# Window attention and two feed-forward layers: chunk 1's first unit is handled ahead of the copies of chunk 0's sums, and softmax work moves to other steps

## The chip, the cores and the metric

The kernel runs on one core of a Trainium2 chip. The metric is device time in microseconds (us) of one execution, as the median of several. Five engines work side by side and wait for one another by semaphores: TensorE (PE in the rows; PEld is its weight loads) multiplies, VectorE (DVE), ScalarE (ACT) and GpSimd (POOL) work element by element, and SyncE (SP) starts most DMAs.

## The reference, cut to what matters

```python
w = softmax(weight_gen)                     # over 7 taps, for 8 heads at each of 2 x 4096 tokens
out = einsum('bshk,bskhg->bshg', w, x_unf)  # each token: 7 rows of x, weighted per head of 24
h = out.reshape(8192, 192) @ w_in1          # 192 x 2048
g = h * cos(h);  y = g @ w_out1             # 2048 x 192
h2 = y @ w_in2;  g2 = maximum(0.01 * h2, h2)
return g2 @ w_out2
```

Products are in fp32 quality: every operand is split in a high part (rounded by a copy) and a low part (the rest, by a subtraction), and TensorE sums high x high, high x low and low x high.

## The kernel before

The 8192 tokens are worked in 16 chunks of 512. Iteration `i` (0 to 16) computes the first layer of chunk `i` and the second layer of chunk `i - 1`, in 18 steps. The 2048 hidden columns are taken in 8 units of 256 for each layer: `FIRST_UNITS` stand in steps 0 to 7, `SECOND_UNITS` in steps 8, 9, 10, 11, 12, 14, 15 and 17. Steps 13 and 16 have no unit. In this text unit (i, q) is unit q (0 to 15) of iteration i; q 0 to 12 stand in the step of the same number, q 13 in step 14, q 14 in step 15 and q 15 in step 17 (so q 8 to 12 are steps 8 to 12).

Of one unit of the first layer: TensorE fills a PSUM slot (`slot0` to `slot2`, by step modulo 3); ScalarE rounds it to whole turns (`whole`, L791); VectorE makes the fraction (L1017); ScalarE takes the sine (L832); VectorE multiplies (L1043, `g_ready`); ScalarE copies the high part (`g_hi`, L732, `hi_ready`); VectorE subtracts (`g_lo`, L919, `lo_ready`); and TensorE adds the unit's second product to `acc_a` and `acc_b`. Of a unit of the second layer ScalarE makes `gate` from the slot (L795) and `g_hi`, and VectorE only `g_lo`.

TensorE's order is fixed: `both_products(i, q, j, r)` fills unit (i, q) and, three units behind, sums unit (j, r). Its first ten half matmuls are of the filling alone; then it waits for `lo_ready` of the unit to be summed. The filling of unit (i, 0) reads the chunk's input: `x1_a_hi` in the first two terms, `x1_a_lo` in the third, `x1_b` (both halves) in the fourth, and `x1_up` in the fifth. It is done beside the sum of unit (i - 1, 13).

ScalarE and VectorE each run `step_of(i, step)` for every step. In a step the high part and the low part of the unit of the step before are taken (`pending_high`, `pending_low`). In step 16 `split_high` and `split_low` make the next chunk's input from `x_raw_a` and `x_raw_b`: `x1_a_hi` (L743) and `x1_b`'s upper half (L745) on ScalarE, `x1_a_lo` (L931) and `x1_b`'s lower half (L934) on VectorE; `x1_up` is a copy on ScalarE (L755) up to chunk 2 and on GpSimd (L659) from chunk 3 on. After the last unit of a layer the sums are copied out of PSUM: in step 0 of iteration 1 for chunk 0, otherwise in step 9, by `leave_mid_a` on ScalarE (L759) and `leave_mid_b` on VectorE (fold L948, `mid_b` L953).

Between these stand the attention of the next chunk (on VectorE in steps 7 to 11, `ATT_AT`) and the softmax of chunks further ahead. The softmax of a group of chunks is max, subtract, exponentials, sum, guard, invert, multiply: the exponentials are on ScalarE (`EXP_AT`, L855), the rest on VectorE (`SOFT_AT`, L1068 to L1083). Exponentials and sine need different tables, so each `exponentials` and each `load_sine` in the loop comes with an `ACT_TABLE_LOAD`. They stand in iterations 1, 3 and 5.

GpSimd makes the low parts of the second layer's weights once: `in_a_lo` in two pieces (L686), `in_b_lo` (L691) and `out_hi_lo` in eight (L697). It starts on them when the multiply of softmax part 2 is done (`soft_count(2, "multiply")`).

## Time and profile before

| what | before |
|---|---|
| median of 3 runs | 1150.26 us (1150.2 to 1150.3) |
| profiled execution, its own time | 1151.76 us |
| span of the profiled execution, first to last instruction | 1150.0 us |
| TensorE busy | 1132.5 us (98%) |
| VectorE busy | 934.6 us (81%) |
| ScalarE busy | 724.9 us (63%) |
| GpSimd busy | 87.1 us (8%) |
| granted TensorE clock, mean | 0.997 |

The profile lists the instructions of one execution with start and length, what ended each engine's idle time, and a chain of work followed back from the last instruction. A number in brackets behind a row is idle time ahead of it, and the name behind the arrow is what ended it. Since matmuls are pipelined, one is 0.39 us long while the next starts 0.23 us behind it.

### The profile page before, as it was taken

Reading aid. Unit: us, or ns where it says so; the run is one execution under the profiler, and the core shown is the slowest. Engines: PE = TensorE matmul, PEld = TensorE weight load, DVE = VectorE, ACT = ScalarE, POOL = GpSimd, SP = SyncE. Lnnn points to the kernel's source line nnn. Section 1 sums busy time; section 2 is a strip of 40 time slices with the busy share of each in tenths; the row PEclk is TensorE's granted clock in tenths of the full one; section 3 lists DMA queues with packets and bytes.
Section 4 is the critical chain, followed back from the end, with each engine's and each line's share of the span. In section 5 each row is a group of like instructions: output and inputs, shape, how many; then the busy total and the mean of one; then the engine's idle time right before and its main releaser. Section 6 shows DMA issues by size and latency. Waiting matters only on the chain.

```text
span 1150.0 us, 22937 instructions
## 1 busy us (share of the span) xinstructions
PE 1132.5 (98%) x9766; PEld 996.1 (87%) x9766; DVE 934.6 (81%) x913; ACT 724.9 (63%) x775; POOL 87.1 (8%) x80
## 2 busy tenths in 40 slices
PE   7999999999999999999999999999999999999998
PEld 5778989988888888899998989988888898898976
DVE  7989798888979889697896978969798796978543
ACT  5666774766747666575665757566575665757544
POOL 5870000000000000000000000000000000000000
PEclk9999999999999999999999999999999999999999
DMA  9760201103011020201102011020201102010001
GB/s 257 203 129 1 63 2 32 45 1 77 1 37 41 1 76 1 54 24 31 47 1 76 1 36 42 4 74 1 47 31 30 48 1 77 1 37 7 1 15 29
DMA packets 85262, 48.41 MB, mean 42 GB/s; under 512 B 58156, under 2 KB 78762, under 8 KB 84776
## 3 DMA queue, kind: packets, MB, share of 16 engines
q1 hardware_dynamic: 80712, 41.70, 14.1%
q0 software_dynamic: 4448, 5.24, 2.5%
q8 instruction: 77, 1.26, 0.4%
q14 instruction: 25, 0.20, 0.1%
HBM read 35.12 MB, written 11.80 MB: 41 GB/s over the span
## 4 chain that ended last, share of the span: by engine, by line
PE 89%; DVE 4%; ACT 1%; issue 1%; ACTq 0%; DVEq 0%
PE slot L1200 41%; PE acc_a L1200 28%; PE acc_b L1200 18%; DVE g_lo L919 1%; DVE prods L327 0%; DVE prods L318 0%; ACT g_hi L732 0%; DVE gate L1017 0%; PE acc_b L1173 0%; ACT gate L795 0%; ACT L855 0%; PE acc_b L1174 0%; PE acc_a L1166 0%; PE acc_a L1165 0%; ACT taps_w L855 0%
## 5 line engine op out<-in xcount | busy, mean ns | idle before, releaser
L1200 PE MATMUL acc_a<-g_hi,out_hi_lo 64*128 64x512 f32 x2000 | 699.0, 390 | 0.0
L919 DVE TENSOR_TENSOR g_lo<-gate,g_hi 128x1024 fp32r<-128x1024 f32 x252 | 309.2, 1227 | 119.0 <-ACT g_hi L732 118.5
L1200 PE MATMUL acc_b<-g_hi,out_hi_lo 64*128 64x512 f32 x1000 | 389.6, 390 | 5.7 <-DVE g_lo L919 3.0
L1200 PEld LDWEIGHTS acc_a<-g_hi,out_hi_lo 64*128 64x128 f32 x2000 | 370.0, 185 | 26.6
L1200 PE MATMUL acc_a<-g_lo,out_hi_lo 64*128 64x512 f32 x1000 | 387.9, 388 | 0.0
L1200 PE MATMUL acc_b<-g_lo,out_hi_lo 64*128 64x512 f32 x1000 | 387.6, 388 | 0.0
L732 ACT ACTIVATE g_hi<-gate 128x1024 fp32r<-128x1024 f32 x252 | 267.3, 1061 | 97.4 <-PE acc_b L1200 78.0
L1200 PE MATMUL slot<-x_a_hi,in_a_lo 64*128 64x512 f32 x1024 | 301.8, 390 | 1.3 <-DVE g_lo L919 0.6
L1200 PE MATMUL slot<-x_a_lo,in_a_hi 64*128 64x512 f32 x1024 | 300.9, 388 | 0.4 <-DVE x_a_lo L938 0.4
L1200 PE MATMUL slot<-x_b,in_b_hi 64*128 64x512 f32 x1024 | 300.9, 388 | 0.2 <-DVE x_b L941 0.2
L1200 PE MATMUL slot<-x_a_hi,in_a_hi 64*128 64x512 f32 x1024 | 300.7, 388 | 0.0
L795 ACT ACTIVATE gate<-slot 128x1024 f32<-128x1024 f32 x128 | 130.8, 1022 | 125.4 <-PE slot L1200 99.0
L1200 PEld LDWEIGHTS acc_b<-g_hi,out_hi_lo 64*128 64x128 f32 x1000 | 184.9, 185 | 24.8 <-issue 8.9
L1200 PEld LDWEIGHTS acc_a<-g_lo,out_hi_lo 64*128 64x128 f32 x1000 | 185.3, 185 | 12.1
L1200 PEld LDWEIGHTS acc_b<-g_lo,out_hi_lo 64*128 64x128 f32 x1000 | 185.0, 185 | 10.4
L1017 DVE SCALAR_TENSOR_TENSOR gate<-slot,whole 128x1024 f32<-128x1024 f32 x127 | 155.1, 1221 | 46.8 <-ACT whole L791 46.1
L791 ACT ACTIVATE whole<-slot 128x1024 int32<-128x1024 f32 x127 | 130.1, 1024 | 72.7 <-PE slot L1200 72.7
L1200 PEld LDWEIGHTS slot<-x_a_hi,in_a_lo 64*128 64x128 f32 x1024 | 145.9, 185 | 17.4 <-PE slot L1200 2.9
L1200 PEld LDWEIGHTS slot<-x_a_lo,in_a_hi 64*128 64x128 f32 x1024 | 146.1, 185 | 13.2 <-DVE x_a_lo L938 0.8
L1200 PEld LDWEIGHTS slot<-x_b,in_b_hi 64*128 64x128 f32 x1024 | 146.1, 185 | 13.0 <-DVE x_b L941 1.0
L1200 PEld LDWEIGHTS slot<-x_a_hi,in_a_hi 64*128 64x128 f32 x1024 | 146.1, 185 | 12.0
L1043 DVE SCALAR_TENSOR_TENSOR gate<-slot,gate 128x1024 f32<-128x1024 f32 x124 | 151.6, 1222 | 6.0 <-ACT gate L832 4.1
(110 smaller groups left out, 1023.0 us busy)
## 6 DMA issues: line engine op xcount, KB each, us to landing
x_win<-in_x SPq DMA_DIRECT2D x14, 960.0 KB, 4.7
x_columns<-prods SPq DMA_DIRECT2D x56, 96.0 KB, 2.0
out<-turned_a SPq DMA_DIRECT2D x240, 16.0 KB, 1.5
x_raw_a<-x_columns SPq DMA_DIRECT2D x14, 256.0 KB, 2.8
out<-turned_b SPq DMA_DIRECT2D x120, 16.0 KB, 1.5
result<-x_columns SPq DMA_DIRECT2D x14, 128.0 KB, 3.0
out_raw<-in_moe_w_out SPq DMA_DIRECT2D x3, 512.0 KB, 8.6
out_hi_lo<-in_moe_w_out POOLq DMA_DIRECT2D x2, 768.0 KB, 10.7
```

What stands on the lines that cost most here:

```text
L732: nc.scalar.activation(g_hi[:, q % 2, :], result_of(i, q), ACT.Copy)\
L791: nc.scalar.activation(whole[:, q % 2, :], slot, ACT.Identity, bias=0.25)\
L795: nc.scalar.activation(gate[:, q % 2, :], slot, ACT.Prelu, alpha=0.01)\
L919: nc.vector.tensor_tensor(g_lo[:, q % 2, :], result_of(i - b, q), g_hi[:, q % 2, :].bitcast(FP32), ALU.subtract)\
L1017: nc.vector.scalar_tensor_tensor(gate[:, q % 2, :], slot, 0.25, whole[:, q % 2, :], ALU.add, ALU.subtract)\
L1043: nc.vector.scalar_tensor_tensor(result_of(i, q), slot, RADIANS, gate[:, q % 2, :], ALU.mult, ALU.mult)\
L1200: return nc.tensor.matmul(to, w[rows, :], x[rows, :], start=start, stop=stop)
```

## The change

- `SOFT_AT` and `EXP_STEP`, `SINE_STEP`: max and subtract of a group stand together in step 12 (before: step 8 of iteration 1, and steps 13 and 14 of iterations 2 and 4). The exponentials stand in step 13 (before 10) and the sine's table load in step 14 (before 12) of iterations 1, 3 and 5. Sum, guard and invert stand in step 16 (before: sum in 13, guard and invert in 14), and the multiply in step 17 (before 16).
- The sum, guard, invert and multiply of part 2 move from step 9 of iteration 0 to step 0 of iteration 1, behind the fraction of unit (1, 0).
- In step 0 of iteration 1, VectorE's product of unit (1, 0) comes ahead of fold and `mid_b`, and its `g_lo` right behind them, ahead of the fraction of unit (1, 1). ScalarE's `g_hi` of unit (1, 0) comes ahead of `mid_a` and of `whole` of unit (1, 1).
- GpSimd starts on the second layer's weights when `g_lo` of unit (1, 0) is done.

```diff
--- before.py
+++ after.py
@@ -432,18 +432,16 @@
             yield (b_lows(W1.in_b_lo, cols), b_lows(W1.in_b_lo_raw, cols),
                    b_pairs(W1.in_b_hi, cols).bitcast(FP32))
 
-        EXP_STEP, SINE_STEP = 10, 12
+        EXP_STEP, SINE_STEP = 13, 14
         HEAD_ROWS, SOFT_ROWS = [[slice(a * J * heads, b * J * heads) for a, b in chunks]
                                 for chunks in (SOFT_HEADS, SOFT_CHUNKS)]
 
 
-        SOFT_AT = {(0, 9): [(2, part) for part in TAIL_PARTS]}
+        SOFT_AT = {}
         for n, (begin, end) in enumerate(((1, 1), (2, 3), (4, 5)), 2):
-            SOFT_AT[begin, 8 if n == 2 else 13] = [(n, "max")]
-            SOFT_AT.setdefault((begin, 8 if n == 2 else 14), []).append((n, "subtract"))
-            SOFT_AT[end, 13] = [(n + 1, "sum")]
-            SOFT_AT[end, 14] = [(n + 1, "guard"), (n + 1, "invert")]
-            SOFT_AT[end, 16] = [(n + 1, "multiply")]
+            SOFT_AT[begin, 12] = [(n, "max"), (n, "subtract")]
+            SOFT_AT[end, INPUT_STEP] = [(n + 1, "sum"), (n + 1, "guard"), (n + 1, "invert")]
+            SOFT_AT[end, INPUT_STEP + 1] = [(n + 1, "multiply")]
         EXP_AT, SINE_AT = [[(i, step) for i in (1, 3, 5)] for step in (EXP_STEP, SINE_STEP)]
 
         def softmax_operands(rows):
@@ -679,7 +677,7 @@
                 .then_inc(w2_hi_loaded[2], 16)
 
 
-            pool.wait_ge(soft, soft_count(2, "multiply"))
+            pool.wait_ge(lo_ready, unit(1, 0) + 1)
             pool.wait_ge(w2_loaded[0], 16)
             pool.wait_ge(w2_hi_loaded[0], 16)
             for cols in W2_PIECES:
@@ -734,7 +732,7 @@
 
             def pending_high(i, step):
                 b, prev = back(step, 1)
-                if is_unit(i - b, prev):
+                if (i, step) != (1, 1) and is_unit(i - b, prev):
                     high_part(i - b, UNITS.index(prev))
 
             def split_high(i, step, chunk):
@@ -831,6 +829,9 @@
                     act.wait_ge(fraction, first_units(i, q))
                     nc.scalar.activation(gate[:, q % 2, :], gate[:, q % 2, :], ACT.Sin,
                                          scale=TURN).then_inc(cos_ready, 1)
+                if (i, step) == (1, 0):
+
+                    high_part(1, 0)
                 j = first_out(i, step)
                 if j is not None:
                     act.wait_ge(summed, unit(j, 7) + 1)
@@ -901,9 +902,21 @@
 
         @block.vector
         def _(dve):
+            def product(i, q):
+                slot = slots[UNITS[q] % SLOTS][:, :, :].rearrange("p a n -> p (a n)")
+                dve.wait_ge(cos_ready, first_units(i, q))
+                nc.vector.scalar_tensor_tensor(result_of(i, q), slot, RADIANS, gate[:, q % 2, :],
+                                               ALU.mult, ALU.mult).then_inc(g_ready, 1)
+
+            def low_part(i, q):
+                dve.wait_ge(hi_ready, unit(i, q) + 1)
+                nc.vector.tensor_tensor(g_lo[:, q % 2, :], result_of(i, q),
+                                        g_hi[:, q % 2, :].bitcast(FP32), ALU.subtract)\
+                    .then_inc(lo_ready, 1)
+
             def pending_low(i, step):
                 b, prev = back(step, 1)
-                if is_unit(i - b, prev):
+                if (i, step) != (1, 1) and is_unit(i - b, prev):
                     q = UNITS.index(prev)
                     if unit(i - b, q) == 0:
                         dve.wait_ge(unit_act, 3)
@@ -915,10 +928,7 @@
                                                 g_hi[:, 0, N:].bitcast(FP32), ALU.subtract)\
                             .then_inc(lo_ready, 1)
                         return
-                    dve.wait_ge(hi_ready, unit(i - b, q) + 1)
-                    nc.vector.tensor_tensor(g_lo[:, q % 2, :], result_of(i - b, q),
-                                            g_hi[:, q % 2, :].bitcast(FP32), ALU.subtract)\
-                        .then_inc(lo_ready, 1)
+                    low_part(i - b, q)
 
             def split_low(step, chunk):
                 slot = slots[step % SLOTS]
@@ -1023,6 +1033,12 @@
                     for instruction in of_chunk_1[ATT_POOL + 1:]:
                         instruction()
                 pending_low(i, step)
+                if (i, step) == (1, 0):
+
+
+                    for part in TAIL_PARTS:
+                        softmax(2, part)
+                    product(1, 0)
                 j = first_out(i, step)
                 if j is not None:
                     if j >= 1:
@@ -1038,11 +1054,10 @@
                         nc.vector.scalar_tensor_tensor(result_of(i, q)[:, cols], slot[:, cols], RADIANS,
                                                        gate[:, 0, cols], ALU.mult, ALU.mult)\
                             .then_inc(done, 1)
-                elif in_first:
-                    dve.wait_ge(cos_ready, first_units(i, q))
-                    nc.vector.scalar_tensor_tensor(result_of(i, q), slot, RADIANS,
-                                                   gate[:, q % 2, :], ALU.mult, ALU.mult)\
-                        .then_inc(g_ready, 1)
+                elif in_first and (i, step) != (1, 0):
+                    product(i, q)
+                if (i, step) == (1, 0):
+                    low_part(1, 0)
                 if i < LAST:
                     split_second_low(i, step)
                 if step == TURN_STEP and i >= 2:
```

VectorE at the start of iteration 1, before. The softmax rows are part 2's, `slot0` holds unit (1, 0) and `slot1` unit (1, 1):

```order
L1074 TENSOR_REDUCE scratch<-taps_w 128x32
L1077 TENSOR_SCALAR scratch<-scratch 128x32
L1080 RECIPROCAL scratch<-scratch 128x32
L1083 TENSOR_TENSOR taps_w<-taps_w,scratch 128x224
L1017 SCALAR_TENSOR_TENSOR gate<-slot0,whole 128x1024
L948 COPY fold<-acc_b 64x512
L953 TENSOR_TENSOR mid_b<-acc_b,fold 64x512
L1043 SCALAR_TENSOR_TENSOR gate<-slot0,gate 128x1024
L1017 SCALAR_TENSOR_TENSOR gate<-slot1,whole 128x1024
L919 TENSOR_TENSOR g_lo<-gate,g_hi 128x1024
L1043 SCALAR_TENSOR_TENSOR gate<-slot1,gate 128x1024
```

The same place now (the fraction is L1027, the product L908, `g_lo` L913):

```order
L1027 SCALAR_TENSOR_TENSOR gate<-slot0,whole 128x1024
L1089 TENSOR_REDUCE scratch<-taps_w 128x32
L1092 TENSOR_SCALAR scratch<-scratch 128x32
L1095 RECIPROCAL scratch<-scratch 128x32
L1098 TENSOR_TENSOR taps_w<-taps_w,scratch 128x224
L908 SCALAR_TENSOR_TENSOR gate<-slot0,gate 128x1024
L958 COPY fold<-acc_b 64x512
L963 TENSOR_TENSOR mid_b<-acc_b,fold 64x512
L913 TENSOR_TENSOR g_lo<-gate,g_hi 128x1024
L1027 SCALAR_TENSOR_TENSOR gate<-slot1,whole 128x1024
L908 SCALAR_TENSOR_TENSOR gate<-slot1,gate 128x1024
```

The fraction moved ahead of the four softmax rows, the product ahead of the fold, and `g_lo` ahead of the next unit's fraction.

ScalarE at the same place, before; `g_hi` is that of unit (1, 0):

```order
L791 ACTIVATE whole<-slot0 128x1024
L832 ACTIVATE gate<-gate 128x1024
L759 ACTIVATE mid_a<-acc_a 128x512
L791 ACTIVATE whole<-slot1 128x1024
L732 ACTIVATE g_hi<-gate 128x1024
```

And now:

```order
L789 ACTIVATE whole<-slot0 128x1024
L830 ACTIVATE gate<-gate 128x1024
L730 ACTIVATE g_hi<-gate 128x1024
L757 ACTIVATE mid_a<-acc_a 128x512
L789 ACTIVATE whole<-slot1 128x1024
```

`g_hi` moved ahead of `mid_a` and of the next unit's `whole`.

ScalarE in iteration 3, before, from `gate` of unit (3, 11) on. `taps_w` is the exponentials, `spare` the sine's table load, the three `g_hi` are those of units (3, 10), (3, 11) and (3, 12):

```order
L795 ACTIVATE gate<-slot2 128x1024
L855 ACT_TABLE_LOAD
L855 ACTIVATE taps_w<-taps_w 128x1120
L732 ACTIVATE g_hi<-gate 128x1024
L795 ACTIVATE gate<-slot0 128x1024
L732 ACTIVATE g_hi<-gate 128x1024
L850 ACT_TABLE_LOAD
L850 ACTIVATE spare<-ident 1x1
L732 ACTIVATE g_hi<-gate 128x1024
```

And now, from `gate` of unit (3, 12) on; the two `g_hi` in one row are those of (3, 11) and (3, 12), the one behind `spare` is that of (3, 13):

```order
L793 ACTIVATE gate<-slot0 128x1024
L730 ACTIVATE g_hi<-gate 128x1024 x2
L793 ACTIVATE gate<-slot2 128x1024
L856 ACT_TABLE_LOAD
L856 ACTIVATE taps_w<-taps_w 128x1120
L793 ACTIVATE gate<-slot0 128x1024
L851 ACT_TABLE_LOAD
L851 ACTIVATE spare<-ident 1x1
L730 ACTIVATE g_hi<-gate 128x1024
L741 ACTIVATE x1_a_hi<-x_raw_a 128x512
L743 ACTIVATE x1_b<-result 64x512
```

Both table loads and the exponentials moved from ahead of `g_hi` of (3, 10) and (3, 12) to ahead of `g_hi` of (3, 13), behind which stands the next chunk's input.

## Rows read from the trace of the kernel before

**Rows 1.** The page: busy time by engine (first line), and the chain that ended last.
```profile
PE 1132.5 (98%) x9766; PEld 996.1 (87%) x9766; DVE 934.6 (81%) x913; ACT 724.9 (63%) x775; POOL 87.1 (8%) x80
...
PE 89%; DVE 4%; ACT 1%; issue 1%; ACTq 0%; DVEq 0%
```

**Rows 2.** Timeline of TensorE: start, length, instruction, idle before and what ended it.
```profile
74.74 0.50 PE L1200 MATMUL acc_b<-g_hi,out_hi_lo 64*128 64x512 f32 x1 [1.77 <-DVE g_lo L919]
...
85.12 0.39 PE L1200 MATMUL acc_b<-g_hi,out_hi_lo 64*128 64x512 f32 x1
...
111.86 0.47 PE L1200 MATMUL acc_b<-g_hi,out_hi_lo 64*128 64x512 f32 x1 [0.71 <-DVE mid_b L953]
...
263.87 0.50 PE L1200 MATMUL acc_b<-g_hi,out_hi_lo 64*128 64x512 f32 x1 [0.38 <-DVE g_lo L919]
```

**Rows 3.** Waits of TensorE: in total, how many times, the longest.
```profile
PE acc_b L1200 <- DVE g_lo L919: 3.0, 4, 1.8
```

**Rows 4.** Windows: length, busy times, granted clock, DMA share, GB/s.
```profile
75.10:78.60 3.50, 3.50 (x20) 2.76 (x18) 3.50 (x4) 2.12 (x2) 3.50 (x4) 0.51 0.01 2
```

**Rows 5.** Timeline of VectorE at the start of iteration 1.
```profile
64.98 0.38 DVE L1074 TENSOR_REDUCE scratch<-taps_w 128x32 f32<-128x224 f32 x1
...
66.31 1.22 DVE L1017 SCALAR_TENSOR_TENSOR gate<-slot,whole 128x1024 f32<-128x1024 f32 x1
68.56 0.69 DVE L948 COPY fold<-acc_b 64x512 f32<-64x512 f32 x1 [1.03 <-PE acc_b L1200]
69.29 0.68 DVE L953 TENSOR_TENSOR mid_b<-acc_b,fold 64x512 f32<-64x512 f32 x1
...
72.23 2.46 DVE L919 TENSOR_TENSOR g_lo<-gate,g_hi 128x1024 fp32r<-128x1024 f32 x1
```

**Rows 6.** Timeline of ScalarE at the start of iteration 1.
```profile
64.25 1.03 ACT L791 ACTIVATE whole<-slot 128x1024 int32<-128x1024 f32 x1 [0.44 <-PE slot L1200]
67.57 1.06 ACT L832 ACTIVATE gate<-gate 128x1024 f32<-128x1024 f32 x1 [2.29 <-DVE gate L1017]
69.46 0.60 ACT L759 ACTIVATE mid_a<-acc_a 128x512 f32<-128x512 f32 x1 [0.83 <-PE acc_a L1200]
69.95 1.02 ACT L791 ACTIVATE whole<-slot 128x1024 int32<-128x1024 f32 x1
```

**Rows 7.** Timeline of GpSimd on the second layer's weights.
```profile
66.49 4.76 POOL L686 TENSOR_TENSOR in_a_lo<-in_a_raw,in_a_hi 128x1024 fp32r<-128x1024 f32 x2 [5.08 <-DVE taps_w L1083]
71.22 2.39 POOL L691 TENSOR_TENSOR in_b_lo<-in_b_lo_raw,in_b_hi 128x1024 fp32r<-128x1024 f32 x1
```

**Rows 8.** Timeline of TensorE: filling of unit (2, 0), then of unit (3, 0).
```profile
133.11 0.40 PE L1200 MATMUL slot<-x_b,in_b_hi 64*128 64x512 f32 x2
...
202.02 0.42 PE L1200 MATMUL slot<-x_a_lo,in_a_hi 64*128 64x512 f32 x2
202.25 0.42 PE L1200 MATMUL slot<-x_b,in_b_hi 64*128 64x512 f32 x2
```

**Rows 9.** Timeline of ScalarE: iteration 1, iteration 2 (no exponentials), iteration 3.
```profile
124.04 1.06 ACT L732 ACTIVATE g_hi<-gate 128x1024 fp32r<-128x1024 f32 x1 [0.69 <-PE acc_b L1200]
...
193.25 1.06 ACT L732 ACTIVATE g_hi<-gate 128x1024 fp32r<-128x1024 f32 x1 [3.24 <-PE acc_b L1200]
...
199.04 0.62 ACT L745 ACTIVATE x_b<-result 64x512 fp32r<-64x512 f32 x1
...
255.49 1.14 ACT L855 ACTIVATE taps_w<-taps_w 128x1120 f32<-128x1120 f32 x1
...
260.93 1.28 ACT L850 ACT_TABLE_LOAD   x1
262.22 0.20 ACT L850 ACTIVATE spare<-ident 1x1 f32<-1x1 f32 x1
```

**Rows 10.** Timeline of VectorE: the input of chunk 3, in iteration 2.
```profile
200.00 1.10 DVE L931 TENSOR_TENSOR x_a_lo<-x_raw_a,x_a_hi 128x512 fp32r<-128x512 f32 x1
201.13 0.68 DVE L934 TENSOR_TENSOR x_b<-result,x_b 64x512 fp32r<-64x512 f32 x1
```

## The prediction

> **What bounds the kernel now.** The page comes first: TensorE is busy for 1132.5 of 1150.0 us, and 89% of the chain that ended last is its matmuls [rows 1]. So an edit elsewhere is worth what it takes from TensorE's waits, or adds to them. The second view is TensorE's timeline, read for idle time. A matmul of 0.39 us is followed by the next after 0.23 [rows 8], so a wait shown as idle costs 0.16 more than its figure. Behind the start-up four waits are within the change's reach: 1.77 ahead of the sum of unit (1, 0), 0.71 ahead of that of (1, 8), and 0.38 ahead of (3, 11) and again ahead of (5, 11) [rows 2, 3]. They cost 1.93, 0.87 and twice 0.54. The third view is the clock: in the 3.5 us behind the longest wait the granted clock was half [rows 4]. Its price is read from the sums: (1, 0) starts at 74.74 and (1, 2) at 85.12 [rows 2], 10.38 for two units. A unit otherwise takes 4.32, since the filling of (2, 0) and that of (3, 0) lie 69.14 apart for 16 units [rows 8]. So half clock cost 1.75. All that the change can win is 1.93 + 1.75 + 0.87 + 1.08 = 5.6 us, 0.5%.
>
> **The start of iteration 1.** I follow the new order with old lengths; what follows without a wait starts 0.07 to 0.10 before its predecessor's shown end, and a semaphore takes 0.03 to 0.05. `whole` of (1, 0) ends at 65.28 as before [rows 6]. VectorE's fraction now comes first: 65.31 to 66.53. The four softmax instructions took from 64.98 to about 66.40 [rows 5], 1.42 us, so now 66.45 to 67.87; the sine (1.06 [rows 6]) ends at 67.63, hidden by them. The product runs from 67.78 to 68.99, fold and `mid_b` (0.69 and 0.68 [rows 5]) to 70.32. ScalarE's `g_hi` runs from 69.03 to 70.09, and VectorE's `g_lo` from 70.25 to 71.47. TensorE asks for it at 74.74 - 1.93 = 72.81. So the wait is gone with 1.3 us to spare, and the half clock behind it with it. `mid_a` and `mid_b` are 0.5 and 0.35 us later, which nobody waits for before 72.8.
>
> What is late next is unit (1, 1). `mid_a` and `whole` of (1, 1) stand behind `g_hi`: `whole` ends at 71.51 (before 70.97 [rows 6]). Fraction to 72.76, sine to 73.86, product to 75.11, `g_hi` to 76.21, `g_lo` from 76.24 to 77.46. TensorE wants to sum it at 72.81 + 4.31 = 77.12 and starts at 77.51, a new wait of 0.39. The sum of (1, 2) then starts at 81.82 instead of 85.12: **3.3 us won**. Behind that VectorE needs some 3.5 us a unit (a fraction, a `g_lo`, a product) against TensorE's 4.31, and catches up.
>
> **GpSimd behind it.** Its first three pieces take 2.37, 2.37 and 2.39 us [rows 7]. The trace shows what they do to VectorE: `g_lo` of (1, 0), asked for at 72.23, took 2.46 instead of 1.22, as it began only about when GpSimd's `in_b_lo` ended (71.22 + 2.39 = 73.61, less 0.14); fraction and product, which read PSUM, were not slowed [rows 5, 7]. Now GpSimd starts at 71.56, so the third piece would start at 71.56 + 4.73 = 76.29, and the second lets go at about 76.20. VectorE asks for `g_lo` of (1, 1) at 76.24, between the two. I take it that it goes first, by 0.05 us, and GpSimd waits. The weights end some 6 us later than before, far ahead of unit (1, 8), the first to need them; the eight short pieces of `out_hi_lo` can hold up a `g_lo` by at most one piece, against a lead that has grown again.
>
> The Trainium skill says the same of this pair (SBUF — State Buffer, Who interferes with whom): whichever of the two starts first holds the shared ports for its whole instruction and the other blocks fully, and a VectorE instruction with one SBUF input is not touched. The rows above agree. It makes the whole stake a full piece.
>
> **Softmax out of step 8.** Without max and subtract ahead of it, chunk 1's fold waits for TensorE alone, and the sum of (1, 8) no longer for `mid_b`: 0.87 won. In step 12 of iterations 1, 2 and 4 the two lie ahead of a `g_lo` whose `g_hi` comes later anyway: nothing.
>
> **Exponentials out of step 10.** The waits at (3, 11) and (5, 11) came from ScalarE's table load and exponentials ahead of `g_hi` of (i, 10), with the attention's last steps pushed back behind it. Iteration 2 has no exponentials and no wait there. So 2 x 0.54 = 1.08 won.
>
> **Exponentials in step 13.** Here lies the price. I take iteration 2 as the pattern and put the new instructions in. `g_hi` of (i, 12) cannot start before TensorE ends a sum: 193.25 [rows 9]. Then come `gate` (to 195.24), table load 1.28, exponentials 1.14 (to 197.66), `gate` of the next unit (to 198.60), table load 1.28 and 0.20 (to 200.11) [rows 9], `g_hi` of (i, 13) (200.16 to 201.22), `x1_a_hi`, and `x1_b` (to 202.30, where the pattern has 199.66). On VectorE `g_lo` of (i, 13) runs from 201.25 to 202.48, `x1_a_lo` to 203.08, `x1_b` to 203.79. TensorE wants `x1_b` in the fourth term of the filling of (i + 1, 0), at 202.25 [rows 8]: in the pattern it was there at 201.81 [rows 10], 0.44 ahead. Now TensorE starts it at 203.84, **1.6 us late**. GpSimd's copy of `x1_up` starts at about the moment when VectorE asks for `x1_a_lo`, as in the pattern, where that took 1.10 instead of 0.68 [rows 10]: 0.4 more, 2.0 in all, in iterations 3 and 5. Without the copy it would be 1.6, and I take 2.0, since one of the two must wait. In iteration 1 the same chain starts at 124.04 [rows 9]; its exponentials are shorter (672 elements of 1120, an estimate of 0.75 us) and there is no GpSimd copy: `x1_b` at 124.04 + 10.54 - 0.39 = 134.19, wanted at 133.11 [rows 8]: 1.1 late.
>
> **Sums in steps 16 and 17.** In the pattern's lengths they fill VectorE's idle time behind `g_lo` of (i, 14) and make the first fraction of the next iteration about 1 us late, against a lead of over 1.5 us at the sum that needs it: nothing. Cover gone, it would be some tenths.
>
> **Sum.** -3.3 - 0.87 - 1.08 + 1.1 + 2 x 2.0 = -0.15 us. Against the profiled execution's 1151.76 that is 1151.6; the median of the runs is 1150.26, so **1150.1 us**. Why the profiled execution is 1.5 above the median no row says. If its half-clock stretch is not in the other runs, the gain there is 1.75 smaller and the time 1151.9, still no change that a measurement can tell (0.2% or 2.3 us).
>
> **Rivals.**
> 1. *GpSimd gets the ports first (slower).* VectorE's request at 76.24 and GpSimd's next piece at 76.29 are 0.05 apart, and each time is a sum of some eight lengths known to 0.01 or 0.02. From a request 0.05 later on, `g_lo` of (1, 1) waits for the third piece: 76.29 + 2.39 - 0.14 + 1.22 = 79.76. TensorE stands for 2.7 us, more than at the old wait, and half clock follows as in rows 4: the sum of (1, 2) starts at 85.9 instead of 81.8. 4.1 us more, 1154.2; without half clock 1152.4.
> 2. *A new wait halves the clock.* The waits of 2.0 us in iterations 3 and 5 are as long as the old one of 1.93, behind which the clock fell, but parted in two (for `x1_a_lo` and for `x1_b`) with matmuls between; the wait of 0.87 did not lower it. 1.75 for each: 1151.9 or 1153.6. The Trainium skill (TensorE: Matmul & The Clock Gate, HAM oscillation) lays a fall to idle gaps longer than any here; by that rule neither the old wait nor the new ones would cost clock, which rows 4 contradict for the old.
> 3. *The waits in steps 16 stay small (faster).* If ScalarE's chain were shorter than its parts, or the input's low parts came ahead of VectorE's `g_lo`, the price would be a third: 1145 to 1147.
> 4. *The change doesn't take effect at (1, 0).* Were something else late there, fold above all, the 3.3 us would stay: 1153.4. The fold needs only 69.6 against 72.8; small.
>
> **How the numbers follow.** Forecast 0.47, rival 1 0.24, rival 2 0.12 (two thirds of it one fall, within 0.2%), rival 3 0.14, rival 4 0.03. The forecast's own range is 1148.5 to 1152.0. Faster by over 0.2%: 0.15. Slower by over 0.2%: rival 1 nearly whole, part of 2, rival 4 and the forecast's upper edge, 0.34. Within: 0.51. The range leaves out the far half of rival 3 and rival 1's upper end: 1147.0 to 1154.5.
>
> **What would show it.** Right: no idle ahead of the sum of (1, 0) and no half clock behind it; 0.4 us ahead of (1, 1); no waits at (1, 8), (3, 11), (5, 11); waits named after `x_a_lo` and `x_b` of the input, 1.1 us in iteration 1 and 2.0 in 3 and 5. Rival 1: `g_lo` of (1, 1) shown with over 3 us, and GpSimd's pieces unbroken. Rival 2: half clock near 134, 270 or 410. Wrong: waits at the input under 0.5 us, or a wait elsewhere in iterations 1 to 5.

## The result, and the profile of the changed kernel

| what | before | changed |
|---|---|---|
| median of 20 runs each, side by side | 1150.53 us (1149.69 to 1151.78) | 1152.39 us (1151.08 to 1155.47) |
| ratio | | 1.0015, interval 1.0009 to 1.0022 |
| profiled execution, its own time | 1151.76 us | 1151.52 us |
| span | 1150.0 us | 1149.7 us |

The changed kernel is slower by 1.86 us. That is inside the band of 0.2% and inside the range, but it can be told from no change, and the forecast was a gain of 0.15. The two profiled executions alone would say that it is 0.24 faster. Both facts have to be explained. Three executions of the old kernel beside the experiments were disturbed (1414.57, 2335.8 and 6518.82 us) and stand in no median or range below.

In the listings below the lines have moved: the matmul is L1215, the fraction L1027, the product L908, `g_lo` L913, fold and `mid_b` L958 and L963, `x_a_lo` and `x_b` of the input L941 and L944, the table loads L856 and L851. The page shows the same bound as before (busy time by engine, then the chain that ended last):

```profile
PE 1132.5 (99%) x9766; PEld 940.0 (82%) x9766; DVE 936.7 (81%) x913; ACT 723.7 (63%) x775; POOL 87.5 (8%) x80
...
PE 88%; DVE 4%; ACT 2%; issue 2%; ACTq 0%; DVEq 0%
```

Four lines of TensorE's waits (total, times, longest), where [rows 3] had 3.0, 4, 1.8 for `g_lo`:

```profile
PE slot L1215 <- DVE x_a_lo L941: 2.2, 3, 0.9
...
PE acc_b L1215 <- DVE g_lo L913: 1.2, 3, 0.5
...
PE slot L1215 <- DVE x_b L944: 0.6, 3, 0.2
PE acc_b L1215 <- DVE mid_b L963: 0.6, 1, 0.6
```

TensorE's timeline has where they stand: the sum of (1, 0), now without a wait; the sums of (1, 1), (1, 4) and (1, 8); the input of chunk 2, and that of chunk 4:

```profile
71.75 0.39 PE L1215 MATMUL acc_b<-g_hi,out_hi_lo 64*128 64x512 f32 x1
...
76.53 0.49 PE L1215 MATMUL acc_b<-g_hi,out_hi_lo 64*128 64x512 f32 x1 [0.30 <-DVE g_lo L913]
...
90.11 0.50 PE L1215 MATMUL acc_b<-g_hi,out_hi_lo 64*128 64x512 f32 x1 [0.37 <-DVE g_lo L913]
...
108.25 0.46 PE L1215 MATMUL acc_b<-g_hi,out_hi_lo 64*128 64x512 f32 x1 [0.58 <-DVE mid_b L963]
...
129.81 0.50 PE L1215 MATMUL slot<-x_a_lo,in_a_hi 64*128 64x512 f32 x2 [0.38 <-DVE x_a_lo L941]
130.52 0.50 PE L1215 MATMUL slot<-x_b,in_b_hi 64*128 64x512 f32 x2 [0.21 <-DVE x_b L944]
...
270.06 0.51 PE L1215 MATMUL slot<-x_a_lo,in_a_hi 64*128 64x512 f32 x2 [0.94 <-DVE x_a_lo L941]
270.77 0.50 PE L1215 MATMUL slot<-x_b,in_b_hi 64*128 64x512 f32 x2 [0.21 <-DVE x_b L944]
```

From start to start, less the 0.23 of a matmul, these cost 0.45, 0.53, 0.73, 0.54 + 0.48 and 1.10 + 0.48; chunk 6 repeats chunk 4 with 1.57. The waits at (3, 11) and (5, 11) are gone. The clock stayed full where [rows 4] had 0.51 (window: length, busy times, granted clock, DMA share, GB/s):

```profile
70.00:73.50 3.50, 3.50 (x34) 2.87 (x32) 2.37 (x3) 2.21 (x3) 2.89 (x2) 1.00 1.11 171
```

VectorE's timeline at the start of iteration 1 answers [rows 5]: `g_lo` of (1, 0) takes 1.21 where it took 2.46, and that of (1, 1) 1.29.

```profile
64.26 1.23 DVE L1027 SCALAR_TENSOR_TENSOR gate<-slot,whole 128x1024 f32<-128x1024 f32 x1 [0.25 <-ACT whole L789]
...
66.73 1.22 DVE L908 SCALAR_TENSOR_TENSOR gate<-slot,gate 128x1024 f32<-128x1024 f32 x1
...
69.31 1.21 DVE L913 TENSOR_TENSOR g_lo<-gate,g_hi 128x1024 fp32r<-128x1024 f32 x1
...
72.83 1.23 DVE L908 SCALAR_TENSOR_TENSOR gate<-slot,gate 128x1024 f32<-128x1024 f32 x1 [1.13 <-ACT gate L830]
...
75.18 1.29 DVE L913 TENSOR_TENSOR g_lo<-gate,g_hi 128x1024 fp32r<-128x1024 f32 x1
```

**Where the time went.** The same fillings of a slot, set side by side in the two traces, give the balance. A profiled execution differs from another before the change begins: the filling that starts at 24.11 in the old kernel starts at 23.06 in the new one, where nothing was changed. Less this 1.05, the new kernel is ahead (-) or behind (+):

| stretch | forecast | measured |
|---|---|---|
| (1, 0) and (1, 1), with the half clock | -3.3 | -3.10 |
| (1, 4) | 0 | +0.65 |
| (1, 8) | -0.87 | -0.12 |
| input of chunk 2 | +1.1 | +1.07 |
| iterations 3 and 5 together | +2.92 | +2.40 |
| the rest | 0 | -0.12 |
| sum | -0.15 | +0.78 |

So in this pair the change costs 0.8 and not nothing. Another 1.1 us lies between this pair and the medians. A part of it is the half clock at (1, 0), which this profile of the old kernel had in full and many of its executions have not, as the experiments show. How large that part is stays open.

### The profile page after: what moved, and what is told of

Its sections match the earlier page's. It is cut to its first block, busy times and chain, and to the rows that moved or that the text cites. A ratio compares the mean times of both kernels' runs of the same rounds, so it can differ in the third digit from the quotient of the medians.

```text
span 1149.7 us, 22937 instructions
## 1 busy us (share of the span) xinstructions
PE 1132.5 (99%) x9766; PEld 940.0 (82%) x9766; DVE 936.7 (81%) x913; ACT 723.7 (63%) x775; POOL 87.5 (8%) x80
## 4 chain that ended last, share of the span: by engine, by line
PE 88%; DVE 4%; ACT 2%; issue 2%; ACTq 0%; DVEq 0%
PE slot L1215 41%; PE acc_a L1215 27%; PE acc_b L1215 18%; DVE g_lo L913 2%; DVE gate L1027 1%; ACT gate L793 0%; ACT L851 0%; DVE prods L318 0%; PE acc_b L1188 0%; ACT g_hi L730 0%; ACT taps_w L856 0%; DVE x_a_lo L941 0%; PE acc_a L1181 0%; PE acc_b L1189 0%; PE acc_a L1180 0%
## 5 line engine op out<-in xcount | busy, mean ns | idle before, releaser
L1215 PE MATMUL acc_a<-g_hi,out_hi_lo 64*128 64x512 f32 x2000 | 697.1, 388 | 0.0
L913 DVE TENSOR_TENSOR g_lo<-gate,g_hi 128x1024 fp32r<-128x1024 f32 x252 | 309.9, 1230 | 124.4 <-ACT g_hi L730 124.2
L1215 PEld LDWEIGHTS acc_a<-g_hi,out_hi_lo 64*128 64x128 f32 x2000 | 368.6, 184 | 36.0
L1215 PE MATMUL acc_b<-g_hi,out_hi_lo 64*128 64x512 f32 x1000 | 388.6, 389 | 3.8 <-issue 2.0
L1215 PE MATMUL acc_a<-g_lo,out_hi_lo 64*128 64x512 f32 x1000 | 387.0, 387 | 0.0
L1215 PE MATMUL acc_b<-g_lo,out_hi_lo 64*128 64x512 f32 x1000 | 386.9, 387 | 0.0
L1215 PE MATMUL slot<-x_a_lo,in_a_hi 64*128 64x512 f32 x1024 | 296.6, 387 | 2.2 <-DVE x_a_lo L941 2.2
L1215 PE MATMUL slot<-x_a_hi,in_a_lo 64*128 64x512 f32 x1024 | 297.7, 389 | 1.0 <-DVE g_lo L913 0.7
L1215 PE MATMUL slot<-x_b,in_b_hi 64*128 64x512 f32 x1024 | 296.7, 388 | 0.9 <-DVE x_b L944 0.6
L1215 PE MATMUL slot<-x_a_hi,in_a_hi 64*128 64x512 f32 x1024 | 296.3, 387 | 0.0
L1215 PEld LDWEIGHTS acc_b<-g_hi,out_hi_lo 64*128 64x128 f32 x1000 | 184.2, 184 | 28.4 <-issue 9.0
L1215 PEld LDWEIGHTS acc_a<-g_lo,out_hi_lo 64*128 64x128 f32 x1000 | 184.4, 184 | 17.5
L1215 PEld LDWEIGHTS acc_b<-g_lo,out_hi_lo 64*128 64x128 f32 x1000 | 184.4, 184 | 16.6
L1027 DVE SCALAR_TENSOR_TENSOR gate<-slot,whole 128x1024 f32<-128x1024 f32 x127 | 155.1, 1221 | 41.1 <-ACT whole L789 40.3
L1215 PEld LDWEIGHTS slot<-x_a_hi,in_a_lo 64*128 64x128 f32 x1024 | 142.2, 184 | 23.5 <-PE slot L1215 2.9
L1215 PEld LDWEIGHTS slot<-x_a_lo,in_a_hi 64*128 64x128 f32 x1024 | 142.1, 184 | 21.9 <-DVE x_a_lo L941 3.5
L1215 PEld LDWEIGHTS slot<-x_b,in_b_hi 64*128 64x128 f32 x1024 | 141.9, 184 | 20.9 <-DVE x_b L944 1.6
L1215 PEld LDWEIGHTS slot<-x_a_hi,in_a_hi 64*128 64x128 f32 x1024 | 142.2, 184 | 17.9
L908 DVE SCALAR_TENSOR_TENSOR gate<-slot,gate 128x1024 f32<-128x1024 f32 x124 | 151.6, 1223 | 6.0 <-ACT gate L830 4.4
```

Of the source, the lines that this page charges most:

```text
L908: nc.vector.scalar_tensor_tensor(result_of(i, q), slot, RADIANS, gate[:, q % 2, :], ALU.mult, ALU.mult).then_inc(g_ready, 1)
L913: nc.vector.tensor_tensor(g_lo[:, q % 2, :], result_of(i, q), g_hi[:, q % 2, :].bitcast(FP32), ALU.subtract)\
L1027: nc.vector.scalar_tensor_tensor(gate[:, q % 2, :], slot, 0.25, whole[:, q % 2, :], ALU.add, ALU.subtract)\
L1215: return nc.tensor.matmul(to, w[rows, :], x[rows, :], start=start, stop=stop)
```

## Experiments

Each median below stands beside runs of the kernel before on the same chip. The experiments were spread over four chips, so two of them are best compared by how far each is from the kernel before.

### The kernel before, again

> The kernel before, unchanged, for its spread. Theory A (half clock behind the wait of 1.93 us at unit (1, 0) comes only in some executions, since the clock's fall depends on how the wait lies in time): the clock of its executions takes several values, those with the fall are about 1.75 us longer, and the profile shows the fall at 75 us or doesn't. Then the start part of the change wins 1.5 to 1.9 us in the median, not the 3.1 us that the two profiles show. Theory B (the fall comes in every execution): all executions have the clock 0.997, and the 1.9 us by which the median of the changed kernel is longer must come from the changed kernel alone. Ratio 1.000 in both.

Measured: 1149.86 us as the median of ten executions (1149.54 to 1150.49), ratio 0.9994 (0.9985 to 1.0003). Its profile again has the wait at (1, 0), 1.98, and half clock behind it (TensorE's timeline, then the window behind):

```profile
73.38 0.49 PE L1200 MATMUL acc_b<-g_hi,out_hi_lo 64*128 64x512 f32 x1 [1.81 <-DVE g_lo L919]
```

```profile
74.00:77.50 3.50, 3.50 (x20) 2.80 (x18) 3.50 (x4) 2.12 (x2) 3.50 (x3) 0.53 0.01 2
```

But six of its ten executions had a mean clock of 1.000, three 0.999, one 0.998. Over all 99 executions of the kernel before that stood beside the experiments, 47 had 1.000, with a median of 1149.70 us; 32 had 0.999 (1150.32), 6 had 0.998 (1150.68) and 14 had 0.997 (1150.75). The median of all is 1150.14. The first profile, at 0.997, is like the last 14.

What these means stand for can be read from the traces. One stretch of 3.4 us at half clock takes 1.7 of 1150 us, or 0.0015 of the mean. A mean of 1.000 thus has no such stretch, this second profile (0.999) has one, and the first profile (0.997) has two. Its other one lies in the start-up, ahead of all that the change touches, and the changed kernel's profile (0.998) has one there too. (Windows of the first profile, then of the changed kernel; the second is 5 us long, so its mean is above half.)

```profile
34.20:37.60 3.40, 3.40 (x19) 3.28 (x18) 3.40 (x4) 2.11 (x3) 3.40 (x4) 0.50 1.09 292
```

```profile
31.00:36.00 5.00, 3.77 (x20) 3.53 (x22) 5.00 (x5) 1.61 (x3) 5.00 (x4) 0.66 0.92 279
```

So the half clock comes in a part of the executions only, and a mean of 0.999 does not say at which place. All in all the lower clocks put the median 0.4 above that of the executions at 1.000 (0.3 to 0.7 on the four chips), and those at 0.997 are only 1.05 longer than those at 1.000, where two stretches at 1.75 would make 3.5. The two profiles of the old kernel show one more thing. Of the 1.8 us between them (1151.76 and 1149.98) 1.4 is there before unit (1, 0), from the start-up, and both have the half clock at (1, 0).

### The softmax part alone

```diff
 (kernel before)
-        EXP_STEP, SINE_STEP = 10, 12
+        EXP_STEP, SINE_STEP = 13, 14
 and the new lines of SOFT_AT for the groups 2 to 4
```

> The kernel before with the new steps of the softmax work alone (max and subtract in 12, exponentials in 13, sine's table load in 14, sum, guard, invert in 16, multiply in 17); the start of iteration 1 and GpSimd as before. If the waits at the chunk input are a property of this part alone: new waits for x_a_lo and x_b of 1.05 us in iteration 1 and 1.6 us in iterations 3 and 5 (4.2 in all), against 0.87 + 0.54 + 0.54 won: 2.3 us over the kernel before, ratio 1.0020. The rival, that the later end of the start part makes them: waits under 0.5 us each, ratio 0.999 or less.

Measured: 1152.36 us (1151.39 to 1154.98), ratio 1.0016 (1.0005 to 1.0026). The input waits are the changed kernel's to 0.02, here that of chunk 4:

```profile
272.72 0.50 PE L1198 MATMUL slot<-x_a_lo,in_a_hi 64*128 64x512 f32 x2 [0.93 <-DVE x_a_lo L929]
273.44 0.49 PE L1198 MATMUL slot<-x_b,in_b_hi 64*128 64x512 f32 x2 [0.22 <-DVE x_b L932]
```

The waits at (1, 8), (3, 11) and (5, 11) are gone, with the old start kept. So the softmax part alone costs as much as the whole change, and within the intervals the start brings the median nothing. The profiled execution is one of three at clock 0.997, which took 1154.25 to 1154.98 where those at 1.000 took 1151.39 to 1152.72 (medians 3.3 apart). It has half clock in the start-up and behind the old wait at (1, 0), and none at the inputs. In the old kernel on the same chip the medians of these two groups are only 1.2 apart. Something there takes most of the clock's price back. The wait at (1, 8), which this kernel lacks, is a candidate, since TensorE would come to it earlier at full clock; no profile of the old kernel at full clock shows it.

### The start alone

```diff
 (changed kernel, with EXP_STEP, SINE_STEP and SOFT_AT of before, the steps of (0, 9) left out)
-        EXP_STEP, SINE_STEP = 13, 14
+        EXP_STEP, SINE_STEP = 10, 12
```

> The changed kernel with the softmax steps of before (exponentials in 10, sine in 12, max and subtract in 8 and so on): the new start of iteration 1 and GpSimd behind g_lo of (1, 0) are left. By the ledger of the two profiles: the wait of 1.93 us (and its half clock where it came) gone, 0.45 at (1, 1) and 0.5 to 0.65 at (1, 4) added, and at (1, 8) about 0.7 us more than the 0.87 of before, since VectorE is late there from GpSimd's pieces and has max and subtract ahead of the fold again. Against an execution of before without half clock that is +0.2 us, against one with it -1.5: ratio 0.999 to 1.000. If GpSimd takes the ports first in a share of the executions, they spread by 2 us and more.

Measured: 1151.17 us (1149.1 to 1153.83), ratio 1.0007 (0.9997 to 1.0017). The start by itself does not win either. It has the waits of the changed kernel at (1, 1) and (1, 4) (0.44 and 0.55), and at (1, 8) 2.48 where before had 0.87 and about 1.6 was expected, with the clock halved behind it (TensorE's timeline, then the window behind):

```profile
109.64 0.76 PE L1217 MATMUL acc_b<-g_hi,out_hi_lo 64*128 64x512 f32 x1 [2.32 <-DVE mid_b L965]
```

```profile
109.80:112.80 3.00, 3.00 (x16) 2.54 (x18) 2.97 (x4) 0.11 (x1) 0.00 (x0) 0.50 0.00 0
```

More than the 1.93 won at (1, 0) comes back by (1, 8): 0.44 + 0.55 + (2.48 - 0.87) = 2.6.

### The exponentials one step earlier

```diff
 (changed kernel)
-        EXP_STEP, SINE_STEP = 13, 14
+        EXP_STEP, SINE_STEP = 12, 13
```

> The changed kernel with the exponentials one step earlier, in step 12, and the sine's table load in step 13. The theory that the waits at the chunk input come from where these stand in ScalarE's idle time: in step 12 ScalarE waits 3.2 us for TensorE ahead of g_hi of (i, 12), and a table load with exponentials is 2.4; in step 13 it waits 1.4, and the sine's load is 1.5. So both are hidden: no wait for x_a_lo or x_b of the input in iterations 3 and 5, at most 0.3 us in iteration 1 (where the exponentials wait for the subtract of the same step), none at (3, 11) and (5, 11). 4.0 us less than the changed kernel: about 1148.4 beside 1152.4, ratio to before 0.9980. The rival, that the table loads cost the same wherever they stand: no change.

Measured: 1147.79 us (1146.94 to 1149.87), ratio 0.9977 (0.9969 to 0.9986). No wait is left at any input. ScalarE's timeline in iteration 3 shows why (changed kernel first, then this one):

```profile
259.92 1.06 ACT L730 ACTIVATE g_hi<-gate 128x1024 fp32r<-128x1024 f32 x1 [3.25 <-PE acc_b L1215]
...
261.91 1.28 ACT L856 ACT_TABLE_LOAD   x1
263.21 1.14 ACT L856 ACTIVATE taps_w<-taps_w 128x1120 f32<-128x1120 f32 x1
...
266.68 1.04 ACT L730 ACTIVATE g_hi<-gate 128x1024 fp32r<-128x1024 f32 x1
```

```profile
255.50 1.28 ACT L856 ACT_TABLE_LOAD   x1
256.79 1.14 ACT L856 ACTIVATE taps_w<-taps_w 128x1120 f32<-128x1120 f32 x1
258.73 1.06 ACT L730 ACTIVATE g_hi<-gate 128x1024 fp32r<-128x1024 f32 x1 [0.79 <-PE acc_b L1215]
...
263.03 1.06 ACT L730 ACTIVATE g_hi<-gate 128x1024 fp32r<-128x1024 f32 x1
```

Ahead of `g_hi` of (3, 12) ScalarE idles for 3.25 us anyway. There the load and the exponentials (2.4 us) fit in, with 0.79 to spare, and `g_hi` of (3, 13) starts 3.65 earlier; 1.19 of that is the lead from iteration 1, which `g_hi` of (3, 12) has too, and 2.46 is the load and the exponentials. The price of the softmax part is thus the one step's choice. What is left are 0.28 each at the first sums of iterations 4 and 6, from the softmax sums in step 16.

### The start of before with that choice

```diff
 (kernel before, with the new SOFT_AT for the groups 2 to 4)
-        EXP_STEP, SINE_STEP = 10, 12
+        EXP_STEP, SINE_STEP = 12, 13
```

> The kernel before with the softmax steps of e3_exp_in_12 (max and subtract in 12, exponentials in 12, sine's load in 13, sum, guard, invert in 16, multiply in 17) and nothing of the change's start: beside e3 this gives the worth of the start part with GpSimd behind it. By the waits in the profiles the start part saves 1.93 us (and half clock in a part of the executions) and gives back 0.45 at (1, 1), 0.55 at (1, 4) and 0.7 at (1, 8): 0.2 us, or about 1.0 with the half clock. So 1148.0 to 1148.8 here, ratio 0.998 to 0.999, beside 1147.8 of e3. If the start part is worth the 3.3 us of the prediction: 1151.

Measured: 1149.0 us (1147.64 to 1150.77), ratio 0.9995 (0.9986 to 1.0004), just above what was expected. This is the last kernel with the new start taken out, so it prices the start. The two kernels stood on different chips, so each is taken against the kernel before beside it: 1.05 faster here and 2.64 there, which makes 1.6 us for the start, where the forecast had 3.3. Its profiled execution had the old wait and full clock (TensorE's timeline, then the window behind):

```profile
73.31 0.50 PE L1198 MATMUL acc_b<-g_hi,out_hi_lo 64*128 64x512 f32 x1 [1.78 <-DVE g_lo L917]
```

```profile
73.90:77.30 3.40, 3.40 (x34) 2.80 (x31) 3.40 (x4) 2.81 (x3) 3.40 (x4) 1.00 0.01 2
```

Behind the start-up it lost 1.94 there, 0.48 at the input of chunk 2 and twice 0.28 at the first sums of iterations 4 and 6, 2.98 in all. The new start has 0.44 + 0.55 + 0.71 and the same twice 0.28, 2.26. At full clock the new start thus wins 0.7 us by the waits, 0.5 of them at the input of chunk 2. The medians of the few executions at 1.000, each against the old kernel's on its chip, say 0.4 (3 and 4 executions). The rest of the 1.6 lies in the executions with a lower clock: at 0.998 the medians are 1150.16 (4 executions) with the old start and 1148.08 (4) with the new one.

### GpSimd released as before

```diff
 (changed kernel)
-            pool.wait_ge(lo_ready, unit(1, 0) + 1)
+            pool.wait_ge(soft, soft_count(2, "multiply"))
```

> The changed kernel with GpSimd started as before, when the multiply of softmax part 2 is done, all else as changed. By the rows of the changed kernel GpSimd's first piece then runs from about 66.9 to 69.3 and the second would start 0.04 us ahead of VectorE's g_lo of (1, 0) at 69.31. If GpSimd has it, g_lo of (1, 0) is 2.4 us later and TensorE waits 1.0 us there; the pieces end 3.6 us earlier, so that the waits at (1, 1), (1, 4) (0.5) and most of that at (1, 8) (0.7) go: 0.5 us less than the changed kernel, ratio to before 1.0010. If VectorE has it, 1.5 us less.

Measured: 1151.18 us (1150.63 to 1153.43), ratio 1.0015 (1.0006 to 1.0024). VectorE had the ports at `g_lo` of (1, 0), as GpSimd's second piece and that `g_lo` show:

```profile
69.15 3.51 POOL L684 TENSOR_TENSOR in_a_lo<-in_a_raw,in_a_hi 128x1024 fp32r<-128x1024 f32 x1
...
69.19 1.21 DVE L913 TENSOR_TENSOR g_lo<-gate,g_hi 128x1024 fp32r<-128x1024 f32 x1
```

The piece is shown 0.04 ahead and yet waited for the whole `g_lo`, so at such a distance the shown starts do not tell who goes first. At (1, 1) GpSimd's first short piece was ahead, by VectorE's and TensorE's timelines:

```profile
75.05 1.76 DVE L913 TENSOR_TENSOR g_lo<-gate,g_hi 128x1024 fp32r<-128x1024 f32 x1
...
76.87 0.50 PE L1215 MATMUL acc_b<-g_hi,out_hi_lo 64*128 64x512 f32 x1 [0.77 <-DVE g_lo L913]
```

(1, 1) costs 0.92 and not 0.45, (1, 4) nothing, (1, 8) 0.47. The sum is 1.39 against 1.71. The 1.5 us less than the changed kernel, expected for this case, did not come: beside the old kernel on its chip this one is 1.06 longer, and the changed kernel 1.09 in its second set.

### GpSimd released by `mid_b`, ahead of `g_lo` of (1, 0)

```diff
 (changed kernel)
-            pool.wait_ge(lo_ready, unit(1, 0) + 1)
+            pool.wait_ge(acc_b_out, 1)
```

> The changed kernel with GpSimd waiting for mid_b of chunk 0 instead of for g_lo of (1, 0): it asks for the ports about 0.1 us behind that g_lo's start and gets them when it ends, some 0.2 us earlier than in the changed kernel, so that its third piece is ahead of g_lo of (1, 1). This makes rival 1 of the prediction come in every execution. If such executions are what lengthens the median of the changed kernel beyond its profile: a wait of 2.3 to 2.7 us at (1, 1), a g_lo of over 3 us there, median 1154 or more (ratio 1.003 to 1.0035), and a smaller spread than the changed kernel's. If the theory is wrong that 0.2 us decide it: the same 0.45 us at (1, 1) and no change beside the changed kernel.

Measured: 1153.55 us (1152.09 to 1155.53), ratio 1.0033 (1.002 to 1.0045). This is rival 1 made to happen, a little under the 1154 expected. The timeline has GpSimd's third piece, VectorE's `g_lo` of (1, 1) and TensorE's sum of it; below it is the window behind:

```profile
75.62 2.37 POOL L689 TENSOR_TENSOR in_b_lo<-in_b_lo_raw,in_b_hi 128x1024 fp32r<-128x1024 f32 x1
...
75.68 3.38 DVE L913 TENSOR_TENSOR g_lo<-gate,g_hi 128x1024 fp32r<-128x1024 f32 x1
...
79.12 0.79 PE L1215 MATMUL acc_b<-g_hi,out_hi_lo 64*128 64x512 f32 x1 [2.39 <-DVE g_lo L913]
```

```profile
79.20:82.20 3.00, 3.00 (x14) 2.43 (x16) 3.00 (x3) 1.89 (x2) 3.00 (x4) 0.50 0.00 0
```

VectorE asked 0.06 later than GpSimd and waited for the whole piece. In the changed kernel VectorE's `g_lo` started at 75.18, 0.16 ahead of GpSimd's third piece, and VectorE was first:

```profile
75.34 3.41 POOL L689 TENSOR_TENSOR in_b_lo<-in_b_lo_raw,in_b_hi 128x1024 fp32r<-128x1024 f32 x1
```

The Trainium skill says this of the pair (SBUF — State Buffer, Who interferes with whom): who issues first has the shared ports for its whole instruction. Both profiles agree.

### GpSimd's short pieces later

```diff
 (changed kernel, ahead of the eight pieces of out_hi_lo)
+            pool.wait_ge(lo_ready, unit(1, 4) + 1)
```

> The changed kernel with the last eight pieces of GpSimd (out_hi_lo) held back until g_lo of (1, 4) is done, about 90 us. If these pieces make the wait of 0.5 us at (1, 4), by holding up the g_lo's of (1, 2), (1, 3) and (1, 4) and x_a_lo by about 0.65 each, it goes; they then fall on the attention's steps, whose products and additions have two inputs in SBUF, and the wait at (1, 8) grows from 0.7 to 1.5 or more. Rival: the wait at (1, 4) comes from the order of VectorE alone and stays.

Measured: 1150.55 us (1150.03 to 1151.75), ratio 1.0006 (0.9997 to 1.0015). The wait at (1, 4) is gone, as it should if the pieces made it. That at (1, 8) was expected to grow and is 0.63, no more than in the changed kernel.

### GpSimd's new wait alone

```diff
 (kernel before)
-            pool.wait_ge(soft, soft_count(2, "multiply"))
+            pool.wait_ge(lo_ready, unit(1, 0) + 1)
```

> The kernel before with one thing of the change: GpSimd waits for g_lo of (1, 0). VectorE's and ScalarE's order at the start of iteration 1 stay. In the kernel before g_lo of (1, 0) lasted 2.46 us because in_b_lo held the ports. If that was 1.2 of the 1.93 us of wait: 0.7 us of wait is left at (1, 0), no half clock, and 0.3 to 0.7 come back at (1, 1) or later: 0.3 to 1.0 us less than before, ratio 0.9992. If the order on VectorE made the wait and not the ports: 1.9 us stay.

Measured: 1151.33 us (1150.26 to 1153.19), ratio 1.0013 (1.0004 to 1.0022), a miss. The first half came as expected: `g_lo` of (1, 0) took 1.23 and its sum waited 0.71, so 1.2 of the old 1.93 was the ports. But then VectorE met GpSimd elsewhere (timelines of GpSimd, VectorE and TensorE):

```profile
78.78 2.40 POOL L691 TENSOR_TENSOR in_b_lo<-in_b_lo_raw,in_b_hi 128x1024 fp32r<-128x1024 f32 x1
...
78.81 3.45 DVE L919 TENSOR_TENSOR g_lo<-gate,g_hi 128x1024 fp32r<-128x1024 f32 x1
...
82.32 0.49 PE L1200 MATMUL acc_b<-g_hi,out_hi_lo 64*128 64x512 f32 x1 [0.39 <-DVE g_lo L919]
...
110.97 0.47 PE L1200 MATMUL acc_b<-g_hi,out_hi_lo 64*128 64x512 f32 x1 [2.29 <-DVE mid_b L953]
```

Here the engine shown 0.03 ahead, GpSimd, did go first, and VectorE lost 2.2 us. TensorE felt 0.54 of that at once; at (1, 8), 30 us later, where TensorE itself was now earlier and VectorE later, the wait grew from 0.87 to 2.44.

### Shorter pieces, and the sums back in step 13

```diff
 (changed kernel, first kernel)
-        PIECE = 1024
+        PIECE = 512
-        EXP_STEP, SINE_STEP = 13, 14
+        EXP_STEP, SINE_STEP = 12, 13
-            pool.wait_ge(lo_ready, unit(1, 0) + 1)
+            pool.wait_ge(soft, soft_count(2, "multiply"))
 (and in the second kernel)
-            SOFT_AT[end, INPUT_STEP] = [(n + 1, "sum"), (n + 1, "guard"), (n + 1, "invert")]
+            SOFT_AT[end, 13] = [(n + 1, "sum")]
+            SOFT_AT[end, INPUT_STEP] = [(n + 1, "guard"), (n + 1, "invert")]
```

> The changed kernel with exponentials in step 12 and the sine's load in 13, GpSimd started as before, and in_a_lo in four pieces of 512 columns instead of two of 1024. No g_lo can then be held up by in_a_lo for more than 1.2 us, which is about TensorE's slack at (1, 0). Expected beside e3_exp_in_12 (1147.8): the waits at (1, 1) and (1, 4) gone or under 0.3 each, (1, 8) under 0.5: 1146.9, ratio to before 0.997. If the start of GpSimd does not matter: as e3_exp_in_12.

> e7_short_pieces with the softmax sum in step 13 instead of 16 (guard, invert and multiply stay in 16 and 17). e3 and e7 show 0.27 us ahead of the first sum of iterations 4 and 6, where VectorE's fold comes late behind sum, guard, invert and multiply. If these cause it, 1.3 us less of them in step 16 removes both waits: 0.5 us less than e7, 1146.1 beside 1146.6. If the fold is late for another reason: no change.

Measured: the first 1146.62 us (1145.47 to 1147.87), ratio 0.9969 (0.9958 to 0.9981); the second **1145.37 us** (1145.07 to 1146.28), ratio 0.9965 (0.9952 to 0.9977). Both beat both kernels. The wait at (1, 4) is gone, as it already was with GpSimd released as before and pieces of 1024; the two edits were not tried apart on the kernel with the exponentials in step 12, so what the short pieces bring by themselves stays open. In the first, 0.39 stayed at (1, 1) (expected under 0.3), 0.41 at (1, 8), 0.20 at the input of chunk 2 and 0.27 each at the first sums of iterations 4 and 6; in the second they are gone, and 0.39 at (1, 1), 0.46 at (1, 8) and 0.18 at the input of chunk 2 are left. The intervals of the two ratios overlap; that the second is better is read from the waits.

### The changed kernel, again

> The changed kernel, unchanged. The ledger of its profile gives 0.8 to 1.3 us over the kernel before where the median of 20 executions gave 1.9. If a share of its executions loses the ports at (1, 1) (e5 shows 2.5 us there): two groups of times, near 1151 and near 1153, and in the profile of one of the second group a g_lo of (1, 1) of 3.4 us. If not: one group, and the rest of the difference lies in how often the clock falls behind the waits at the chunk input.

Measured: 1151.26 us (1150.49 to 1154.12), ratio 1.0014 (1.0005 to 1.0023). Its profile, at clock 1.000, has the same waits to 0.03 and one more of 0.34 at 199.56. The times are one group from 1150.49 to 1152.46 with one execution at 1154.12, not two groups, and nine of the eleven have a clock of 1.000. The half clock is not what makes the changed kernel slow.

## Why the prediction was wrong, step by step

**The start of iteration 1: the walk held.** The old lengths in the new order gave the product at 67.78, `g_lo` of (1, 0) at 70.25 and of (1, 1) at 76.24. Less the 1.05 of the start-up these are 66.73, 69.20 and 75.19; the trace has 66.73, 69.31 and 75.18. The new wait was forecast at 0.39 and is 0.45. VectorE did go first at the ports. In this pair of profiles the step brought 3.10 of 3.3.

**The half clock in the median: the step that failed first.** The prediction took 1.75 of its 3.3 from one stretch of one execution, and subtracted it from a median. Of 99 executions 47 had a mean clock of 1.000, so no such stretch at all, and the lower clocks of the others lengthen the median by 0.4 in all (0.7 on the chip where it is most), the stretch of the start-up included. So of the 1.75 at most that was there to be won. At full clock the wait at (1, 0) costs its 1.93 and no more, as the profile with the old start and the good softmax steps shows. The prediction named this case itself (1151.9). It found the profiled execution 1.5 above the median and no row to say why: 1.4 us of it is the late start-up, by the second profile, which has the same half clock at (1, 0) and took 1149.98. The filling that starts at 24.11 in the first profile starts at 22.66 in the second, and at 22.48 to 23.58 in all thirteen others of this study. The distance to the median thus said nothing of the stretch at (1, 0); only more executions could.

**"A lead that has grown again": the second step that failed.** The prediction let GpSimd's short pieces pass at nothing, since VectorE would have caught up. The two windows of equal length, from behind the sum of (1, 1) to the sum of (1, 8), show that it didn't (first before, then changed; the busy times are of PE, PEld, DVE, ACT and POOL):

```profile
79.40:110.80 31.40, 31.40 (x280) 27.12 (x276) 28.94 (x28) 21.52 (x24) 4.96 (x5) 1.00 0.01 2
```

```profile
75.84:107.28 31.44, 30.77 (x269) 24.77 (x266) 31.30 (x27) 21.95 (x25) 13.14 (x9) 1.00 0.00 1
```

VectorE was idle for 2.5 us there before, and is idle for 0.1 now. Its busy time includes its waits for the ports. The new start put TensorE 3.1 ahead but VectorE only 0.7: its product of (1, 1) stands at 72.83 + 1.05 = 73.88, before at 74.61. And GpSimd's pieces, which come later, now meet more of its two-input instructions:

```profile
78.73 1.79 DVE L913 TENSOR_TENSOR g_lo<-gate,g_hi 128x1024 fp32r<-128x1024 f32 x1
...
82.79 1.93 DVE L913 TENSOR_TENSOR g_lo<-gate,g_hi 128x1024 fp32r<-128x1024 f32 x1
...
85.77 1.35 DVE L1000 TENSOR_TENSOR x_a_lo<-mid_a,x_a_hi 128x512 fp32r<-128x512 f32 x1
...
88.18 1.88 DVE L913 TENSOR_TENSOR g_lo<-gate,g_hi 128x1024 fp32r<-128x1024 f32 x1
```

With 1.22 and 0.68 as their free lengths that is 2.6 us of waiting for the ports. It makes the 0.53 at (1, 4), which goes when the pieces start later. It does not by itself make the 0.73 at (1, 8), which stays at 0.63 then: held back, the pieces still cost VectorE 1.0 us between 89 and 98 (its `g_lo` at 91.89 takes 1.77). How much of the wait at (1, 8) is theirs stays open.

**Softmax out of step 8: right, and the gain taken back.** Max and subtract (1.7 us) no longer delay the fold; alone with the old start, the wait goes. But `mid_b` ends only 2.56 earlier than before on a common clock, and TensorE asks 2.42 earlier. The 0.87 became 0.73 instead of 0. In the start alone it is 2.48, so the removal was worth 1.75, not 0.87: it pays for the new start.

**Exponentials out of step 10: right,** 1.08 won.

**Exponentials in step 13: right in place and kind, 0.9 too dear in all.** Forecast 1.1 and twice 2.0, measured 1.02 and 1.58, 1.57. In iteration 3 the walk, with 0.4 for GpSimd's copy, had the last input 10.99 behind the start of `g_hi` of (3, 12), and TensorE asking for it 9.00 behind. The trace has 270.77 - 259.92 = 10.85, with `x_a_lo` at 1.10 as in [rows 10], and TensorE asking at 269.19, 9.27 behind. The term mis-sized is 0.14 in the chain and 0.27 in the moment of asking, which the pattern of an iteration without delay set too early.

**Sums in steps 16 and 17: nothing, right for this kernel.** When the waits at the inputs go, 0.28 twice comes out from under them.

**The rivals.** Rival 1 is real as a mechanism and to the size (wait forecast 2.7, made 2.54; 1152.4 to 1154.2, made 1153.55), and did not happen in any profile of the changed kernel; whether its two executions above 1154 (1155.47, and 1154.12 among the second set) are such cases stays open. Rival 2, a new wait that halves the clock, was not seen at the inputs in any profile, and at a wait of 2.48 at (1, 8) it was. Rivals 3 and 4 fell. The outcome was near the second case of the forecast, "1.75 smaller and the time 1151.9": 1.3 of waits at (1, 4) and (1, 8) that it had at nothing, less the 0.9 that it had too much at the inputs. That the two nearly cancel is luck.

**The balance at full clock.** Won: 1.93, 1.08 and 0.87 - 0.73. Lost: 0.45, 0.53, 1.02, 1.58 and 1.57. That is +2.0 us. It takes the 0.87 from profiles with half clock at (1, 0); at full clock that wait may be longer, and the balance smaller. The medians at clock 1.000 are 1149.70 before, and 1152.03 and 1151.26 for the two sets of runs of the changed kernel: +2.3 and +1.6. Against the old kernel's ten executions at 1.000 on its own chip (1149.44) the second set is +1.8.
